# Attention and two mixture layers on one core: operands laid out ahead of the kernel, scores a turn ahead, later output stored transposed

## What is computed

```python
for c in range(S // 32):                      # chunks of 32 tokens
    k_ctx = k[:, :, max(0, 32*c - 16):min(S, 32*c + 40)]      # v_ctx likewise
    scores = scale * q_c @ concat([mem_k, k_ctx]).T
    a = exp(scores - max(scores)); a /= sum(a) + 1e-9
    out_c = a @ concat([mem_v, v_ctx])
x = out as [3072 tokens, 512]
x = ((x @ w_a) * (x @ w_b)) @ w_out           # w_a, w_b [512, 1536]
P = exp(x @ w_gate - max); 8 times: rows to sum 1, columns to sum 1, times N/E
out = sum over 8 experts e of P[:, e] * (max(x @ w1[e], 0) @ w2[e])   # w1[e] [512, 1024]
```

## Time and profile before

| | |
|---|---|
| median of 3 runs | 2609.35 us |
| the profiled execution | 2608.89 us; its span 2607.2 us |
| TensorE matmul busy | 2552.3 us, 98% of the span |
| VectorE, ScalarE, GpSimd busy | 1514.6, 992.4, 1611.4 us |
| mean granted clock of TensorE | 0.995 |
| first product of line 1025 | at 145.5 us |
| DMA | 530.4 MB, 190,061 packets, 55,544 of them under 512 B |

### The profile page before, as it was taken

The page is one execution under the profiler, slowest core; times in us unless marked ns, Lnnn a source line. Parts: engine busy times, 40 slices in busy tenths (PEclk is TensorE's granted clock), DMA queues, the critical chain, the costliest instruction groups (busy, mean ns, idle before and its releaser), DMA issues.

```text
span 2607.2 us, 38013 instructions
## 1 busy us (share of the span) xinstructions
PE 2552.3 (98%) x14418; PEld 2102.8 (81%) x14418; DVE 1514.6 (58%) x2293; ACT 992.4 (38%) x1722; POOL 1611.4 (62%) x1329
## 2 busy tenths in 40 slices
PE   7889999999999999999999999999999999999998
PEld 6668878888778888888888888888887888888887
DVE  3554554544666555555566566665666665656665
ACT  4653422322434334433343333333334333333333
POOL 2385410200477777777767777777679677776776
PEclk8899999999999999999999999999999999999999
DMA  9665544334276666666665555545555565455553
GB/s 216 155 223 218 209 167 157 145 146 169 86 270 237 258 234 231 250 253 255 237 252 221 202 209 187 223 179 208 196 201 200 189 214 217 183 210 202 191 221 118
DMA packets 190061, 530.42 MB, mean 203 GB/s; under 512 B 55544, under 2 KB 124088, under 8 KB 170680
## 3 DMA queue, kind: packets, MB, share of 16 engines
q1 hardware_dynamic: 168792, 517.43, 54.1%
q10 hardware_dynamic: 21088, 10.55, 1.6%
HBM read 367.41 MB, written 160.60 MB: 203 GB/s over the span
## 4 chain that ended last, share of the span: by engine, by line
PE 90%; POOL 3%; DVE 2%; issue 2%; ACT 2%; SPq 0%; DMA 0%; ACTq 0%; DVEq 0%; POOLq 0%
PE bank L1025 45%; PE bank L1124 22%; PE bank L1102 19%; POOL X L762 1%; PE bank L933 1%; POOL H L886 1%; PE bank L963 1%; PE bank L987 1%; PE bank L975 0%; ACT X L1361 0%; SPq L621 0%; DVE tmp L1759 0%; DMA W<-w_kept 0%; PE bank L997 0%; PE bank L1002 0%
## 5 line engine op out<-in xcount | busy, mean ns | idle before, releaser
L1025 PE MATMUL bank<-X,W 128*128 128x512 f32 x5550 | 1396.5, 390 | 8.3 <-POOL X L762 2.3
L1025 PEld LDWEIGHTS bank<-X,W 128*128 128x128 f32 x5550 | 1038.7, 188 | 232.6 <-issue 7.2
L886 POOL TENSOR_TENSOR H<-tmp,H 128x512 fp32r<-128x512 f32 x448 | 578.0, 1303 | 309.5 <-ACT H L1571 309.4
L1124 PE MATMUL bank<-H,W2n 128*128 128x512 f32 x2688 | 682.0, 389 | 2.7 <-POOL H L886 2.5
L1834 DVE TENSOR_TENSOR Y<-Y,bank 128x512 f32<-128x512 f32 x752 | 496.7, 682 | 293.7 <-PE bank L1124 293.6
L1124 PEld LDWEIGHTS bank<-H,W2n 128*128 128x128 f32 x2688 | 504.2, 188 | 109.1 <-POOL H L886 3.8
L1571 ACT ACTIVATE H<-tmp 128x512 fp32r<-128x512 f32 x448 | 275.2, 628 | 460.7 <-DVE tmp L1864 236.0
L1102 PE MATMUL bank<-W,hid 128*128 128x512 f32 x1536 | 385.1, 389 | 0.7 <-POOL W L734 0.7
L1102 PEld LDWEIGHTS bank<-W,hid 128*128 128x128 f32 x1536 | 288.2, 188 | 61.0 <-POOL W L734 1.1
L762 POOL TENSOR_TENSOR X<-Y,X 128x1024 fp32r<-128x1024 f32 x30 | 79.6, 2661 | 365.7 <-ACT X L1361 365.6
L1811 DVE SCALAR_TENSOR_TENSOR Y<-bank,gate,Y 128x512 f32<-128x512 f32 x224 | 167.1, 747 | 167.6 <-PE bank L1102 166.5
(11 more groups left out here) (123 smaller groups left out, 2018.8 us busy)
## 6 DMA issues: line engine op xcount, KB each, us to landing
W<-w_kept SPq DMA_DIRECT2D x88, 1792.0 KB, 11.5
W2n<-w2n_kept SPq DMA_DIRECT2D x64, 1536.0 KB, 8.3
w_kept<-W SPq DMA_DIRECT2D x44, 1792.0 KB, 8.2
raw<-in_moe_w_dram SPq DMA_DIRECT2D x64, 512.0 KB, 4.4
w2n_kept<-W SPq DMA_DIRECT2D x32, 1024.0 KB, 8.0
w2n_kept<-tmp SPq DMA_DIRECT2D x64, 512.0 KB, 8.2
W2n<-w2n_kept SPq DMA_DIRECT2D x64, 256.0 KB, 3.0
W<-w_kept SPq DMA_DIRECT2D x12, 1024.0 KB, 9.1
```

The costliest lines, as they stand in the source:

```text
L886: nc.gpsimd.tensor_tensor(H[:, pos, 1], hidden_at(k, pos), H[:, pos, 0].bitcast(F32), ALU.subtract).then_inc(h_lo, 1)
L1025: last = nc.tensor.matmul(into[:, :], W1[:, c % 2, ws, w_slot, kc, :], X[:, pos, xs, kc, :], start=(start and kc == 0 and n == 0), stop=(k ...
L1124: last = nc.tensor.matmul(b_half[pair][half][:, :], W2n[k % 2][:, a, blk, half * P:(half + 1) * P], H[:, h, b, :], start=(q in (0, 5) and ...
```

## The change

1. kernel() lays out K.T and Q.T, with the memory keys in place, as `kq` (12 thirds of 256 queries, [128, 2400]), and the windows of V as `vw` (24 quads, [128, 4 x 4 x 64]). The units, their loads, copies and transposes go; SP loads a third with one DMA, a quad of V with another. The factor SCALE goes from the copy of Q.T into Exp. The window is stored as chunk, memory, rest, so that one Exp covers all.
2. scores(r+1), maxima(r+1) and differences(r+1) come in turn r; there are two sets of banks for scores. maxima, differences and quotients are one instruction for both f. The first pair's operands and the first two weights are prepared from turn G + 2 = 8 on.
3. Pairs 1 and 2 are stored from Y as they stand, transposed; kernel() turns them back. transpose_out and copy_out go; c22 and c21 of all later units are in bank 7.
4. At the change of block, GpSimd runs the last operand_lo(3, 0, i) after up_sums(C1 + 1), and VectorE runs accumulate(M1 - 1, 0) inside last_of_pair, before operand_lo(n, of, 5).

```diff
+        KQ = KQ0, KQ1, KQ2, KQ3        # [P, HP * (KTH + QTH)] = [128, 2400] each
+        banks = ctx.enter_context(nc.psum_tensor("banks", [P, 8, 512], F32))
+        b_s, b_pt, b_o, b_ot = (banks[:, 0:2, :], banks[:, 2:4, :]), bank[4], banks[:, 5:7, :], bank[7]
...
+            def load_kq(i):
+                if i >= KS:
+                    sp.wait_ge(a_s, 2 * (i - KS) + 2)
+                at = kq_place(i)
+                if i == 0:
+                    sp.dma_start(KQ[at][0:64, :], kq[i, 0:64, :]).then_inc(s_kq[at], 16)
+                else:
+                    sp.dma_start(KQ[at][:, :], kq[i]).then_inc(s_kq[at], 16)
             def load_v(r):
                 if r >= VS:
                     sp.wait_ge(a_o, r - VS + 1)
+                sp.dma_start(Vw[:, r % VS].rearrange("p c h d -> p (c h d)"), vw[r]).then_inc(s_v[r % VS], 16)
...
+                for i, (j, l) in enumerate(added(q) for q in range(3, NP)):
+                    if i < 3:
+                        sp.wait_ge(z_acc, 12 * (p * V2 - 1) + 2 * i + 6)
+                        sp.dma_start(out_block(p, j, l), y_block(p, j, l)).then_inc(s_out, 16)
+                        continue
+                    for half in range(2):
+                        sp.wait_ge(z_acc, 12 * (p * V2 - 1) + 2 * i + 5 + half)
+                        sp.dma_start(out_block(p, j, l)[:, half], y_block(p, j, l)[:, half]).then_inc(s_out, 16)
+            load_kq(0)
             load_v(0)
+            load_kq(1)
             load_v(1)
             load_v(2)
+            load_kq(2)
+            load_kq(3)
             for r in range(VS, R):
                 load_v(r)
-                if r == G - 1:
+                if r % 2 == 1 and r // 2 + 3 < THIRDS:
+                    load_kq(r // 2 + 3)
+                if r == G + 1:
                     load_up(0)
                     load_up(1)
```

On GpSimd the first pair's up_sums, up_lo, operand_lo and first_sum are spread over turns G + 2 to G + 14, and at the change of block:

```diff
-            for i in range(2, len(X_POOL)):
+            for i in range(2, len(X_POOL) - 1):
                 operand_lo(3, 0, i)
             for u in range(V2 - 1):
                 up_sums(C1 + u + 1)
+                if u == 0:
+                    operand_lo(3, 0, len(X_POOL) - 1)
                 up_lo(C1 + u + 1)
```

TensorE:

```diff
+            scores(0)
             for r in range(R):
-                scores(r)
                 if r > 0:
                     transpose_p(r - 1)
+                if r + 1 < R:
+                    scores(r + 1)
                 if r > 1:
                     transpose_o(r - 2)
-                for unit in QUAD_UNITS[r][:1]:
-                    transposed(unit)
                 if r > 0:
                     weigh_v(r - 1)
-                for unit in QUAD_UNITS[r][1:]:
-                    transposed(unit)
-                    if (u, pos) in OUT_SLOTS:
-                        transpose_out(1, OUT_SLOTS.index((u, pos)), b_gate)
-            for i in range(NG):
-                transpose_out(2, i, bank[OUT_BANKS[i]])
```

ScalarE:

```diff
+            act.dma_start(KQ[kq_place(0)][64:P, :], kq[0, 64:P, :]).then_inc(s_kq_half, 16)
+                nc.scalar.activation(Pr[:, r % 2], Df[:, :, :, :], ACT.Exp, scale=SCALE).then_inc(a_exp, 1)
+            exps(0)
             for r in range(R):
                 if r > 0:
                     copy_pt(r - 1)
                 if r > 1:
                     x_quad(r - 2)
-                exps(r)
+                if r == G + 2:
+                    up_hi(0, (0, 1))
...
+                if r + 1 < R:
+                    exps(r + 1)
```

VectorE:

```diff
+                nc.vector.tensor_reduce(nmax[:, r % 2], b_s[r % 2][:, :, 0:HP * KEYS].rearrange("p f (j n) -> p f j n", j=HP),
+                                        AX.X, ALU.max, negate=True).then_inc(a_mx, 1)
+            maxima(0)
+            differences(0)
             for r in range(R):
-                maxima(r)
-                differences(r)
+                if r + 1 < R:
+                    maxima(r + 1)
+                    differences(r + 1)
                 if r > 0:
-                    denominators(r - 1)
                     quotients(r - 1)
-                if r == R - G + 4:
+                denominators(r)
+                if r == G + 10:
                     operand_lo(0, 0, 3)
-                if r == R - G + 5:
+                if r == G + 12:
                     operand_sum(0, 0, 4)
...
                 operand_sum(n, of, 4)
+                if v + 1 == M1:
+                    accumulate(v, 0)
                 operand_lo(n, of, 5)
                 g_lo(v, 3, 1, 0)
```

More of the change, by code:

```diff
@@ L143, in build @@
         with ExitStack() as first:
-            KT1 = sb("KT1", [P, HP, KCOLS], F32, first)
+            KQ0 = sb("KQ0", [P, KQN], F32, first)
+            KQ1 = sb("KQ1", [P, KQN], F32, first)
         hid1 = sb("hid1", [P, 2, 2, 2, TB], F32R)
@@ L407, in first_use @@
             return BUILDS.index(w) if w in BUILDS else None
-        def loads_v(r):
-            return sum((12, 10, 10, 8, 8, 10)[i % G] for i in range(r % VS, r + 1, VS))
         def edge(r):
@@ L1644, in _ @@
             hidden_hi(M2 - V2 - 1, 6)
-            act.wait_ge(s_out, 16 * 2 * NG)
-            for i in range(NG):
-                copy_out(2, i, bank[OUT_BANKS[i]])
         @block.vector
@@ L2109, with by_dims @@
     from concourse.bass_utils import run_bass_kernel_spmd as _run
+    b, h, s, d = inputs['q'].shape
+    m = inputs['mem_k'].shape[2]
+    hp, keys = h // 2, LEFT + CHUNK + RIGHT + m
+    def by_dims(a):
+        a = a.reshape(b, hp, 2, a.shape[2], d)
+        return _np.ascontiguousarray(a.transpose(0, 2, 4, 1, 3)).reshape(b, 2 * d, hp, a.shape[3])
+    k, mem, q = (by_dims(inputs[name]) for name in ('k', 'mem_k', 'q'))
+    k = _np.concatenate([mem, mem, k, mem], axis=3)
+    parts = []
+    for i in range(s // CHUNK):
+        parts += [k[..., i * CHUNK:(i + 1) * CHUNK], mem]
@@ new lines, with by_rows @@
+    parts.append(k[..., s:])
+    k = _np.concatenate(parts, axis=3)
+    step = 2 * P // CHUNK * (CHUNK + m)
+    thirds = []
+    for i in range(b):
+        for at in range(s // (2 * P)):
+            thirds.append(_np.concatenate([
+                k[i, :, :, at * step:at * step + step + keys - CHUNK - m].reshape(2 * d, -1),
+                q[i, :, :, at * 2 * P:(at + 1) * 2 * P].reshape(2 * d, -1)], axis=1))
+    def by_rows(a):
+        a = a.reshape(b, hp, 2, a.shape[2], d)
+        return _np.ascontiguousarray(a.transpose(0, 2, 3, 1, 4)).reshape(b, 2, a.shape[3], hp * d)
@@ new lines @@
+    v, mem = by_rows(inputs['v']), by_rows(inputs['mem_v'])
+    v = _np.concatenate([mem, mem, v, mem], axis=2)
+    quads = []
+    for i in range(b):
+        for g in range(s // P):
+            chunks = []
+            for at in range(g * P, (g + 1) * P, CHUNK):
+                window = v[i, :, at:at + keys - m]
+                chunk = _np.concatenate([window[:, :CHUNK], mem[i], window[:, CHUNK:]], axis=1)
+                chunks.append(chunk.reshape(2 * keys, hp * d))
+            quads.append(_np.concatenate(chunks, axis=1))
```

441 lines of the change are left out of this document (122 added, 319 removed).

## The result

The kernel after takes **2581.1 us** (median of 4 runs, 2580.05 to 2581.53), before it 2609.61 beside it: the ratio is 0.989, with a 95% interval from 0.9876 to 0.9905. It is faster, by 28.5 us, where I forecast 64 and a range that ended at 2562.

The account below looks back on a forecast made before the run. VectorE was taken to bound the attention's turns at 3.3 us, TensorE the stage of products. Gains of 54.2 + 3.7 + 4.2 + 1.5 = 63.6 us from 2608.9 gave 2545 us, range 2535 to 2562.

Parts of the forecast that it names:

- part 1: Attention: transposes, copies and small transfers removed; first product at 91.3 us instead of 145.5, gain 54.2 us.
- What is then the slowest in a turn?: Attention: VectorE sets the turn at 3.3 us; ScalarE, TensorE, GpSimd and DMA all lie under that.
- the term for TensorE: Attention turn: two batches of small products at 0.79 and two of transposes at 0.59, 2.8 us at full clock.
- VectorE's term: Attention turn: maxima, differences, quotients and smaller instructions, each waiting for the one before, 3.3 us; at the least 3.1.
- The bound for slower turns: Attention: 3.67 us a turn, from the last turns of the kernel before; the gain would be 45.7 us.
- So the loop no longer goes through TensorE: Attention: scores two turns ahead are done at 3.6 us, and VectorE needs them only at 5.2.
- Rival B: Attention: TensorE at half clock is the bound, 4.3 us a turn; 2557 in half the turns, 2569 in all; 14%.
- Rival C: Attention: DMA sets the turn; 2585 if large loads run at 226 GB/s, 2552 at 300; 11%.
- Rival D: Attention: VectorE's merged instructions cost more than a 512-column one; 2556, or 2592 at double; 6%.
- E: Products after the attention: TensorE's clock stays at the lower level, kernel slower than before, 2612 or above; 1%.
- Parts 2 to 4: Outside the attention: gains of 3.7 us for pair 1's output, 4.2 at the end, 1.5 at the change of block.
- 98% on faster: Whole kernel: the chance given to a time lower than before by over 0.2%.

Follow-up runs that it names:

- e5: Kernel after with one product for two pairs of heads in scores and weigh_v, 144 TensorE instructions a turn instead of 272: 2543.57 us, first product at 90.8.
- e4: Kernel after without the loads of queries, keys and values once each buffer is filled, TensorE's instructions the same: 2568.81 us, first product at 116.9.
- e6: Kernel after with both one product for two pairs of heads and loads left out after each buffer's first: 2539.04 us, first product at 84.7.
- e11: Kernel before with one product for two pairs of heads in scores and weigh_v, 128 instructions fewer a turn: 2600.0 us, first product at 137.5.
- e8: Kernel before with the output part of the change alone (pairs 1 and 2 stored transposed): 2601.35 us, ratio 0.9963 to before.
- e7: Kernel after with the two orders at the change of block put back: 2585.53 us, ratio 0.9898 to before.
- e1: Kernel after with scores and weigh_v as 8 wider products each instead of 32, 80 TensorE instructions a turn: 2597.91 us, first product at 143.7.
- e9: Kernel after with 16 products in weigh_v instead of 32, V in blocks beside zeros, output still the reference's: 2576.79 us, ratio 0.986 to before.
- e3: Kernel after with 16 one-column products added to each scores, 64 more TensorE instructions a turn: 2607.36 us, first product at 154.1.

## Why the prediction was wrong in its size

**The failed step is in part 1, "What is then the slowest in a turn?"** I listed VectorE, ScalarE, TensorE, GpSimd and DMA, found all under 3.3 us, and so made VectorE the bound. A sixth resource wasn't in the list: the stream of TensorE's own instructions. A turn has 272 of them, a packet brings 256, and packets came 3.5 us apart at the least, 4.64 in the mean. In its place the runs show a mean turn of (127.4 - 10) / 24 = 4.9 us. Halving the instructions (e5) put the first product at 90.8 us; removing the data (e4) moved it by 10.5 only. With it went the term for TensorE, 2.8 us a turn at full clock: it was busy 3.4 a turn, in part at the low clock.

**VectorE's term was too high, and 90.8 beside my 91.3 is luck in part.** I took 3.3 us a turn and 3.1 as the least. Each instruction cost what I had, 0.65 to 0.69 us. But quotients doesn't read what differences wrote, nor the sum of Exp what quotients wrote, nor maxima what the last small one wrote, and each of the three starts 0.05 to 0.08 us before the one ahead has ended. A turn of e5 in which VectorE doesn't wait goes from 64.74 to 67.77, 3.03 us:

```profile
64.74 0.64 DVE L1440 TENSOR_REDUCE nmax<-banks 128x8 f32<-128x512 f32 x1
65.49 0.69 DVE L1447 TENSOR_TENSOR Df<-banks,nmax 128x512 f32<-128x512 f32 x1
66.13 0.69 DVE L1468 TENSOR_TENSOR On<-banks,rsum 128x512 f32<-128x512 f32 x1
66.74 0.67 DVE L1456 TENSOR_REDUCE esum<-Pr 128x8 f32<-128x512 f32 x1
...
67.77 3.01 DVE L1512 TENSOR_TENSOR X<-Y,X 128x1024 fp32r<-128x1024 f32 x1
```

In e6 the starts of maxima are 2.98 to 2.99 apart in 15 turns of 23. With 2.98 my sum gives 84.0, and e6 came at 84.7; in e5 some 7 us of pauses take the place of what I had too much on VectorE.

**The bound for slower turns was one row.** "The present last turns, with the loop through TensorE still in them, take 3.67": a pause of 0.59 us of the supply was in that turn, and the five last ones took 4.1 in the mean. By that my sum would have given 110 us and a gain of 36. That the loop itself took less than 3.67 is likely from the pause, but no run shows it: in e11 V's landings set these turns. A sign was in the trace of before, though not among the rows: the pauses of 0.59 and 1.15 us inside a batch of weigh_v (129.10, 133.25). The [1.85 <-issue] of the earlier trace rows, which was among them, is not a clean one: it stands at the start of a batch, 105 matmuls after the pause before, and ends 0.10 us after V's last landing at 144.65.

**"So the loop no longer goes through TensorE"** stands as an argument on latencies. It didn't matter: TensorE was late by its own stream, and VectorE waited for it, 30.4 and 18.6 us.

**Rival B** had the low clock right (0.73 to 0.86 from 24 to 120 us) and its price too small to be the cause: in its worst case it gave 2569, and the kernel took 2581. With most of the pauses gone in e5 and the columns unchanged, the clock was at 1.00 from 24 to 72 us. Its part, some 17 us of busy time by the estimate above, came together with the pauses. **Rival C** did not come: large loads ran at up to 435 GB/s (2.25 us slices of e5), above the 414 of the earlier trace rows. **Rival D** fell: 0.65 to 0.69 us an instruction. **E** did not come: the clock is 1.00 in the products.

**Parts 2 to 4** hold, to about 1 us, which is what one trace can tell. Pair 1's transposes 3.7 forecast, 3.7 measured (e8). The end 4.2 forecast, 4.9 measured, by e8 and by after alike; the backlog of stores cost nothing, the upper bound was 5. The change of block 1.5 forecast, 1.1 to 1.8 measured (e7); the gap of 1.50 and VectorE's closed, the one for the weights' Lo part grew from 0.67 to 1.12, and 0.6 for ScalarE's copy of u came in, as "partly handed back" had it.

**The chances.** 98% on faster was right. The range was too narrow because every case in it had a bound from the list of five resources.

## What to carry to other kernels

Count instructions as well as their time. Where a stage runs many small matmuls, compare its instructions per turn with the packets on the instruction queue: one per 256, here about 3.5 us apart at best and later when the DMA engines are full. A pause with releaser "issue" in the middle of a batch, at equal distances in instructions and just behind the landing of a packet, was that supply here, and leaving out the loads didn't remove it (e4); fewer, longer instructions did, for the most part (e5). At the start of a batch look at the landings of its data first: there "issue" stood for V in e11. But look at what the wider form costs: e1 traded the pauses for a low clock, e9 for loads on half the partitions.

## What was not expected of the hardware

- TensorE's instructions came in packets of 16 KB, 256 at a time, at least 3.5 us apart in after and mostly 3.5 to 3.9 without other traffic (e4). TensorE stood still until 0.97 to 1.59 us after a packet's landing, at 17 places in after.
- In e1 the clock was 0.50 for over 100 us although TensorE was busy 24.00 of 24.00 us in its windows. What keeps it low there stays open.
- Matmuls of one column weren't cheap: 30 of them in a row, all on the same 64 rows and 32 columns of the array, took 1.74 us in e3, 58 ns each, at a low clock (the transposes after them took 1.11 us). 64 matmuls of 64 columns spread over eight such parts took 1.18 us there, 18 ns each.
- Loads onto 64 of the 128 partitions moved about half: 218 GB/s in after's first load, two halves one behind the other (3 to 6 us), 405 to 427 from 10 to 22 us, with loads onto all 128.
- An instruction of 1024 columns on VectorE took 3.33 us in after's attention (line 1512) against the 1.69 of the earlier trace rows; GpSimd worked beside it for 2.34 us. Elsewhere in after the same line took 1.21.
